# Small inverse beside the MLP in plain float32: two 94-column matmuls a job, and the split of v read from PSUM

## The reference

```
X = rfft(x, axis=1)                      # x: 4 x 3008 x 256
y = irfft(X * (filt_r + 1j*filt_i)[None], n=3008, axis=1)
x = y.reshape(12032, 256)
g = maximum(x @ moe_w_in, 0) ** 2        # 256 -> 2048
x = g @ moe_w_out                        # 2048 -> 256
gate = x @ moe2_w_gate; val = x @ moe2_w_val   # 256 -> 1536
out = (gate * sigmoid(gate) * val) @ moe2_w_out
```

## Time and profile before

| | |
|---|---|
| median of 3 runs | 2361.15 us (2359.8 to 2363.39) |
| profiled execution, its own time | 2358.64 us |
| its span | 2356.8 us |
| TensorE busy | 2329.5 us, 99% |
| VectorE busy | 1601.1 us, 68% |
| ScalarE busy | 1272.7 us, 54% |
| mean granted TensorE clock | 0.997 |

### The profile page before, as it was taken

The page is one execution under the profiler, slowest core; times in us unless marked ns, Lnnn a source line. Parts: engine busy times, 40 slices in busy tenths (PEclk is TensorE's granted clock), DMA queues, the critical chain, the costliest instruction groups (busy, mean ns, idle before and its releaser), DMA issues.

```text
span 2356.8 us, 31292 instructions
## 1 busy us (share of the span) xinstructions
PE 2329.5 (99%) x10581; PEld 1903.6 (81%) x10581; DVE 1601.1 (68%) x2707; ACT 1272.7 (54%) x2468; POOL 61.2 (3%) x124
## 2 busy tenths in 40 slices
PE   8899999999999999999999999999999999999999
PEld 4688888888888888888888878888888888888887
DVE  3567766677666776566555777777777777777776
ACT  4566656566655665555544445555555555555554
POOL 0100000000000000000000000000000000000000
PEclk9899999999999999999999999999999999999999
DMA  9643433333333333101002101001011011010000
GB/s 270 207 132 96 129 96 107 91 107 112 101 98 99 99 106 122 29 27 42 27 19 72 50 1 36 23 14 36 1 36 36 1 36 36 1 36 28 10 19 18
DMA packets 95423, 153.74 MB, mean 65 GB/s; under 512 B 10080, under 2 KB 48416, under 8 KB 94976
## 3 DMA queue, kind: packets, MB, share of 16 engines
q1 hardware_dynamic: 82112, 132.96, 17.9%
q0 software_dynamic: 13152, 18.78, 3.3%
HBM read 101.89 MB, written 49.81 MB: 64 GB/s over the span
## 4 chain that ended last, share of the span: by engine, by line
PE 96%; DMA 2%; SPq 1%; ACT 1%; issue 1%; DVE 1%; POOL 0%; ACTq 0%; DVEq 0%
PE psum L1450 31%; PE psum L1452 31%; PE psum L1451 31%; PE psum L1552 1%; DMA filt0b<-filt 1%; PE psum L1554 1%; PE psum L1461 1%; DMA B_scratch<-b_out 0%; SPq L562 0%; SPq L557 0%; PE psum L1504 0%; DMA w<-w_full 0%; ACT turned L820 0%; DMA A_scratch<-a_out 0%; ACT z_raw L820 0%
## 5 line engine op out<-in xcount | busy, mean ns | idle before, releaser
L1217 DVE SCALAR_TENSOR_TENSOR prod<-psum,act_out 128x512 f32<-128x512 f32 (+1 forms) x384 | 260.9, 679 | 398.4 <-ACT act_out L917 397.9
L917 ACT ACTIVATE act_out<-psum 128x512 f32<-128x512 f32 (+1 forms) x384 | 226.1, 589 | 461.5 <-PE psum L1452 461.2
L1450 PE MATMUL psum<-g_hi,m_hi 128*128 128x512 f32 (+1 forms) x768 | 305.7, 398 | 2.0 <-ACT z_raw L820 1.8
L1450 PE MATMUL psum<-v_hi,m_hi 128*128 128x512 f32 (+1 forms) x768 | 297.7, 388 | 1.5 <-DVE v_lo L1115 1.5
L1452 PE MATMUL psum<-v_hi,m_lo 128*128 128x512 f32 (+1 forms) x768 | 296.7, 386 | 0.0
L1451 PE MATMUL psum<-v_lo,m_hi 128*128 128x512 f32 (+1 forms) x768 | 296.7, 386 | 0.0
L1452 PE MATMUL psum<-g_hi,m_lo 128*128 128x512 f32 (+1 forms) x768 | 296.5, 386 | 0.0
L1451 PE MATMUL psum<-g_lo,m_hi 128*128 128x512 f32 (+1 forms) x768 | 296.4, 386 | 0.0
L1115 DVE TENSOR_TENSOR g_lo<-prod,g_hi 128x512 fp32r<-128x512 f32 (+1 forms) x408 | 270.6, 663 | 1.1 <-ACT g_hi L820 1.0
L820 ACT ACTIVATE g_hi<-prod 128x512 fp32r<-128x512 f32 (+1 forms) x408 | 248.5, 609 | 0.9 <-DVE prod L1251 0.9
L1450 PE MATMUL psum<-g_hi,m_out 128*128 128x512 f32 (+1 forms) x576 | 226.0, 392 | 0.3 <-DVE g_lo L1115 0.3
(11 more groups left out here) (125 smaller groups left out, 4246.9 us busy)
## 6 DMA issues: line engine op xcount, KB each, us to landing
filt_in<-filt SPq DMA_DIRECT2D x36, 512.0 KB, 3.9
z_scratch<-z_raw SPq DMA_DIRECT2D x23, 512.0 KB, 2.9
b_in<-B_scratch SPq DMA_DIRECT2D x122, 96.0 KB, 2.8
zq_raw<-z_scratch SPq DMA_DIRECT2D x44, 256.0 KB, 3.5
B_scratch<-b_out SPq DMA_DIRECT2D x38, 256.0 KB, 2.1
A_scratch<-a_out SPq DMA_DIRECT2D x50, 192.0 KB, 2.1
x_in<-x SPq DMA_DIRECT2D x48, 192.0 KB, 2.8
a_in<-A_scratch SPq DMA_DIRECT2D x36, 256.0 KB, 3.3
```

Of the source, the lines that this page charges most:

```text
L917: nc.scalar.activation(act_out[n % 2][:, 0:w], psum[:, n % 3, 0:w], ACT.Relu).then_inc(relu_done, 1)
L1217: nc.vector.scalar_tensor_tensor(out=prod[n % 2][:, 0:w], in0=psum[:, n % 3, 0:w], scalar=0.0, in1=act_out[n % 2][:, 0:w], op0=ALU.max, op ...
L1450: nc.tensor.matmul(dst, wh, vh, start=start, stop=False, skip_group_check=True)
```

## The change

The s4 job multiplies b as it was loaded with the table as it is, in plain float32: for each i one instruction with 94 columns. Its output in PSUM is the sum already, so copy_part, add_conv, the rings part and conv, and the splits of b go away; ScalarE's high_v reads PSUM and writes v_hi, VectorE's low_v reads PSUM and v_hi and writes v_lo, in the step of the job. Bank INV is free once v_lo is done. The ring of v holds three tiles instead of two, so a whole group is written at once, and only groups at the ring's end are in two pieces. load_b waits for s4 of two groups back instead of the split of that group, and the job itself waits for b's landing. w4's table is half as large. Tiles behind v in SBUF move by a few KB, and the blocks that hold the gated MLP's input are placed otherwise in the same region.

```diff
-RING = 2 * T
+RING = 3 * T
...
-    w4_full = w4[0:G0].transpose(2, 0, 1, 3)
-    w4 = halves(w4, 0).transpose(1, 3, 2, 0, 4)
+    w4 = w4.transpose(0, 2, 1, 3)
+    w4_full = w4[0:G0].transpose(1, 0, 2, 3)
...
-        b_hi, at = place_ring(at, "b_hi", 2, [ROWS, PAIR, D], F32R)
-        b_lo, at = place_ring(at, "b_lo", 2, [ROWS, PAIR, D], F32R)
-        w4, at = place_ring(at, "w4_", 2, [ROWS, PAIR, 2, Q], F32R)
-        part, at = place_ring(at, "part", 2, [P, GT])
-        conv_region = at
-        conv, at = place_ring(at, "conv", 2, [P, CH, GT])
-        fft_region = at
+        w4, at = place_ring(at, "w4_", 2, [ROWS, PAIR, Q])
...
+        at = fft_region = s4_region + 3 * CH * T * 4
...
-                wait(sp, b_lo_done, g - G0 - 1)
+                if g >= G0 + 2:
+                    sp.wait_ge(s4_done, s4_count(g - 2, CH - 1))
...
-            def high_b(g):
...
-            def copy_part(g, c):
...
-            def high_v(g, c, late):
-                t, col, src, size = v_spans(g)[late]
-                act.wait_ge(conv_done, s4_count(g, c))
-                if t >= 2:
-                    act.wait_ge(h_done, NF1 * (t - 1))
-                copy(v_hi[:, c, col:col + size], conv[g % 2][:, c, src:src + size]).then_inc(v_hi_done, 1)
+            def high_v(g, c):
+                act.wait_ge(s4_done, s4_count(g, c))
+                last = (GT * (g + 1) - 1) // T
+                if last >= 3:
+                    act.wait_ge(h_done, NF1 * (last - 2))
+                for col, lo, size in v_spans(g):
+                    copy(v_hi[:, c, col:col + size], psum[:, INV, lo:lo + size]).then_inc(v_hi_done, 1)
...
-            def low_b(g):
...
-            def add_conv(g, c):
...
+            def low_v(g, c):
+                dve.wait_ge(v_hi_done, v_count(g, c))
+                for col, lo, size in v_spans(g):
+                    low(v_lo[:, c, col:col + size], psum[:, INV, lo:lo + size], v_hi[:, c, col:col + size])\
+                        .then_inc(v_lo_done, 1)
...
                 if last_s4 is not None:
-                    pe.wait_ge(conv_done, s4_count(*last_s4))
+                    pe.wait_ge(v_lo_done, v_count(*last_s4))
...
-                pe.wait_ge(b_lo_done, g - G0 + 1)
+                pe.wait_ge(b_loaded[g % 2], 16 * PAIR * ((g - G0) // 2 + 1))
                 pe.wait_ge(w4_loaded[g % 2], 16 * ((g - G0) // 2 + 1))
                 wait(pe, b_copied, s3_jobs)
-                wait(pe, conv_done, s4_count(g, c) - 1)
-                dst = psum[:, INV, 0:2 * GT].rearrange("p (i h q) -> p i h q", i=PAIR, h=2)
+                pe.wait_ge(v_lo_done, v_count(g, 0) - len(v_spans(g)) if c == 0 else v_count(g, 0))
                 for i in range(PAIR):
-                    bh, bl = b_hi[g % 2][:, i, c * P:(c + 1) * P], b_lo[g % 2][:, i, c * P:(c + 1) * P]
-
-                    nc.tensor.matmul(dst[:, i, :, :], bh, w4[g % 2][:, i, :, :], start=True, stop=False,
-                                     skip_group_check=True)
-                    last = nc.tensor.matmul(dst[:, i, 0, :], bl, w4[g % 2][:, i, 0, :], start=False, stop=True,
-                                            skip_group_check=True)
+                    last = nc.tensor.matmul(psum[:, INV, Q * i:Q * (i + 1)], b_in[g % 2][:, i, c * P:(c + 1) * P],
+                                            w4[g % 2][:, i, :], start=True, stop=True, skip_group_check=True)
                 last.then_inc(s4_done, 1)
```

More of the change, by code:

```diff
@@ L181, in build @@
         b_in, at = place_ring(at, "b_in", 2, [ROWS, PAIR, D])
-        b_hi, at = place_ring(at, "b_hi", 2, [ROWS, PAIR, D], F32R)
-        b_lo, at = place_ring(at, "b_lo", 2, [ROWS, PAIR, D], F32R)
-        w4, at = place_ring(at, "w4_", 2, [ROWS, PAIR, 2, Q], F32R)
-        part, at = place_ring(at, "part", 2, [P, GT])
-        conv_region = at
-        conv, at = place_ring(at, "conv", 2, [P, CH, GT])
-        fft_region = at
+        w4, at = place_ring(at, "w4_", 2, [ROWS, PAIR, Q])
+        warm, at = place(at, "warm", [P, 2])
+        assert at <= s4_region + 3 * CH * T * 4
+        at = fft_region = s4_region + 3 * CH * T * 4
         x_in, at = place_ring(at, "x_in", 4, [QP, PAIR, D])
@@ L225, in build @@
         filt0a, at = place(v_region, "filt0a", [P, FILT0, 2, D])
-        assert at <= conv_region
+        assert at <= fft_region
         filt0b, at = place(a_hi_region, "filt0b", [P, K2 - FILT0, 2, D])
@@ L245, in build @@
         z_lo0, z_end = place(at, "z_lo0", [P, CH, T], F32R)
-        assert z_end <= fft_region
+        assert z_end == fft_region
         last_w = TOKENS - T * PLAIN[1]
@@ L251, in build @@
         a_raw, at = place(at, "a_raw", [P, 2 * CH, PIECE])
-        o_plain0, at = place(at, "o_plain0", [P, T])
-        assert at <= s4_region
+        o_plain0, o_plain0_end = place(at, "o_plain0", [P, T])
         z_in, z_hi, z_lo = [z_in0, z_in1], [z_hi0, z_hi1], [z_lo0, z_lo1]
@@ L259, in build @@
         BLOCK = 4 * T
-        blocks = [list(range(at, m1_end, BLOCK)) + list(range(z_end, fft_region - BLOCK + 1, BLOCK))
+        plain_end = v_region + 8 * BLOCK
+        assert plain_end >= o_plain0_end
+        blocks = [list(range(at, m1_end, BLOCK)) + list(range(plain_end, s4_region - BLOCK + 1, BLOCK))
                   + list(range(m2_end, room - BLOCK + 1, BLOCK)),
-                  list(range(v_region, z_end, BLOCK))]
+                  list(range(v_region, plain_end, BLOCK)) + list(range(s4_region, z_end, BLOCK))]
         zq_hi, zq_raw, zq_lo = [[], []], [[], []], [[], []]
@@ L344, in build @@
         b_copied = sem("b_copied")
-        b_hi_done = sem("b_hi_done")
-        b_lo_done = sem("b_lo_done")
         s4_done = sem("s4_done")
-        part_done = sem("part_done")
-        conv_done = sem("conv_done")
         v_hi_done = sem("v_hi_done")
@@ L455, in v_spans, with v_count, v_tile @@
             lo, hi = GT * g, GT * (g + 1)
[L456 to L466, removed]
+            edge = min(hi, RING * (lo // RING + 1))
+            return [(s % RING, s - lo, e - s) for s, e in ((lo, edge), (edge, hi)) if e > s]
+        def v_count(g, c):
+            if g < G0:
+                return CH
+            return CH * (1 + sum(len(v_spans(h)) for h in range(G0, g))) + (c + 1) * len(v_spans(g))
+        def v_tile(t):
+            return v_count(first_group(t + 1) - 1, CH - 1)
         def m2_at(n):
@@ L667, in load_z @@
                 if t == 0:
-                    sp.wait_ge(v_lo_done, v_count[TILES - 1])
+                    sp.wait_ge(v_lo_done, v_tile(TILES - 1))
                     sp.wait_ge(s4_done, s4_count(GROUPS - 1, CH - 1))
@@ L684, in load_zq @@
                     sp.wait_ge(g_used, STEPS)
-                    sp.wait_ge(conv_done, s4_count(GROUPS - 1, CH - 1))
                 elif k == 1:
@@ L802, in load_w4 @@
                     pool.wait_ge(s4_done, s4_count(g - 2, CH - 1))
-                pool.dma_start(w4[g % 2][:, :, :, :], w4_table[g % PGS, :, :, :, :]).then_inc(w4_loaded[g % 2], 16)
+                pool.dma_start(w4[g % 2][:, :, :], w4_table[g % PGS]).then_inc(w4_loaded[g % 2], 16)
             for u in range(UPS - 2):
@@ L823, in _ @@
             act.wait_ge(warm_ready, 1)
-            nc.scalar.activation(conv[0][:, 0, 0:1], conv[0][:, 0, 1:2], ACT.Sigmoid)
+            nc.scalar.activation(warm[:, 0:1], warm[:, 1:2], ACT.Sigmoid)
             def copy_a0(j):
@@ L882, in high_w_out @@
                 copy(m1_hi[:, W_IN + n, :], m1_raw[:, W_IN + n, :]).then_inc(m1_hi_done, 1)
-            def high_b(g):
[L885 to L888, removed]
-            def copy_part(g, c):
-                act.wait_ge(s4_done, s4_count(g, c))
[L892 to L895, removed]
-            def high_v(g, c, late):
-                t, col, src, size = v_spans(g)[late]
-                act.wait_ge(conv_done, s4_count(g, c))
-                if t >= 2:
-                    act.wait_ge(h_done, NF1 * (t - 1))
-                copy(v_hi[:, c, col:col + size], conv[g % 2][:, c, src:src + size]).then_inc(v_hi_done, 1)
+            def high_v(g, c):
+                act.wait_ge(s4_done, s4_count(g, c))
+                last = (GT * (g + 1) - 1) // T
[3 more added lines that the diff above has]
+                    copy(v_hi[:, c, col:col + size], psum[:, INV, lo:lo + size]).then_inc(v_hi_done, 1)
             def high_m2(w):
@@ L1033, in _ @@
                 if job is not None:
[L1034 to L1042, removed]
+                    high_v(*job)
                 u = s3_at(n)
@@ L1048, in _ @@
                     copy_a(j)
-                g = s4_group_at(n + 2)
-                if g is not None:
-                    high_b(g)
                 if n % 4 == 2 and n // 4 + 1 < W_IN // 2:
@@ L1115, in low @@
                 return nc.vector.tensor_tensor(dst, full, as_f32(hi), ALU.subtract)
-            nc.vector.memset(conv[0][:, 0, 1:2], 0.0).then_inc(warm_ready, 1)
+            nc.vector.memset(warm[:, 1:2], 0.0).then_inc(warm_ready, 1)
```

(12 more changed lines are left out.)

## The result

The changed kernel takes 2337.56 us (2336.49 to 2337.73, 4 runs) against 2361.1; the ratio is 0.9898, 95% interval 0.9881 to 0.9915. It is faster by 1.0%, outside the predicted range. Its profiled execution has a span of 2335.9 us, 20.9 less than before.

A forecast was written before the change was run, and what follows sets the result against it. TensorE, busy 99% of the span, was taken as the bound. Gains of 1.2 us (s4 jobs), 0.6 (start) and 0.2 (other waits) sum to 2.0, so 2361.15 becomes 2359.2 us; range 2353.5 to 2366.

The forecast's parts named there:

- What is costed at nothing: Changed bank release, engine and load waits, and later stages' new addresses: all priced at no time.
- the faster one (2345): Rival in the s4 jobs: loads hide, streaming sets the price at 346 ns a job, 15.4 us less; chance 0.05.
- The price of an s4 job: On TensorE, exposed weight loads set a job's cost: 470 ns instead of 480.
- the 30 ns for the long matmuls to fall back into their rhythm: Part of each s4 job's price on TensorE: some 30 ns lost after its short matmuls, before and after the change.
- the 1.2 us that I counted: Gain on TensorE from 115 s4 jobs not covered by waits for z, 10 ns each.
- The start: Ahead of the first x product: without b_lo, x_lo starts earlier and TensorE's 1.92 us wait shrinks by 0.60 us.
- The waits costed at nothing: Waits for the s4 and s3 bank, h_done, loads of b and w4, and b's landing: covered, no cost.
- my 0.2: Further shrinking of TensorE's 2.55 us of waits in the s4 stage, booked at 0.2 us, bounds 0 and 0.4.
- Draining between formats: Rival: array empties between s4's plain passes and float32r matmuls around them, 43.5 us slower, 2402; chance 0.07.
- loads that don't follow the clock: Rival: s4's plain loads stay at 212 ns at full clock, 34.3 us slower, 2394.7; chance 0.05.
- four loads a matmul: Rival: four passes per s4 matmul, eight loads a job instead of four, 50 us slower, about 2410; chance 0.03.
- the loads hide: Rival in the s4 jobs: streaming, not loads, sets the price, 15.4 us less, 2345; chance 0.05.

The follow-up runs named there:

- e1: Kernel before, s4 untouched, with only the region behind the s4 tiles starting 640 bytes later; 2337.33 us, ratio 0.9906 to the kernel before.
- e2: Changed kernel with the second MLP's weights, and the tiles over and behind them, moved by 1408 bytes to their old remainder; 2358.05 us, ratio 0.9995.
- e3: Changed kernel with only the three zq blocks behind the second MLP's weights moved by 1408 bytes; 2340.89 us, one run.
- e5: Changed kernel with every tile moved by 1408 bytes together, w4_0 laid over z_raw; 2332.75 us in one run, 2336.73 us when repeated.
- e6: Changed kernel with the second MLP's weights, and what lies over and behind them, moved by 512 bytes; 2338.87 us, single run.
- e11: Changed kernel with the second MLP's weights, and what lies over and behind them, moved by 32 bytes; 2359.18 us, single run.
- e4: Changed kernel with everything behind the first MLP's weights moved by 1408 bytes, w4_0 laid over z_raw; 2374.45 us.
- e12: Changed kernel with the first MLP's lo weights and the streamed v_lo and g_lo all moved by 128 bytes; 2352.19 us.
- e14: Changed kernel with only the first MLP's lo weights (m1_lo) moved by 128 bytes; 2349.48 us.
- e7: Changed kernel with the second MLP's weights, and what lies over and behind them, moved by 128 bytes; 2356.85 us, single run.
- e10: Changed kernel with the second MLP's weights, and what lies over and behind them, moved by 64 bytes; 2361.91 us, single run.

## Why the prediction was wrong

**The step that failed** is the last sentence of "What is costed at nothing": "The later stages only get other addresses." I gave it no price and no reason. Other addresses were worth 20.2 of the 20.9 us of the span in the quads alone (e1, e2), and the 1.0 us between z and the quads too: that stretch takes 93.3 to 93.6 us in every profile with the second MLP's weights out of step and 92.4 to 92.6 in every other. None of my rivals held it, and the faster one (2345) expected its gain in the s4 jobs, where none was. The trace of before had the hint: 231.3 ns a matmul in the quads against 226.7 in the first MLP for the same shape at the same clock, a difference that no wait and no instruction explained, and that I did not look at because TensorE counted as busy in both.

**The price of an s4 job held, but for its rhythm.** I had 470 ns after 480. The loads inside a job follow each other as those before did. In the timeline of loads of the changed kernel the row of the four plain loads begins at 1029.06, under the last long matmul; the second of them starts at 1029.283 and the float32r load behind the fourth at 1029.617, so the three exposed ones take 111 ns each, and the float32r load 113:

```profile
1029.06 0.64 PEld L1495 LDWEIGHTS psum<-w,b_in 96*128 96x128 f32 x4
1029.62 0.19 PEld L1396 LDWEIGHTS psum<-g_hi,m_hi 128*128 128x128 f32 x1
1029.73 0.19 PEld L1397 LDWEIGHTS psum<-g_lo,m_hi 128*128 128x128 f32 x1
```

So a plain float32 load at full clock lies within my bounds (106 to 112.5), a little above the 109 I took, and at about half of the 212 ns that it took at the granted clock 0.50. The steps, to be held against the earlier trace rows:

```profile
1027.92 0.39 PE L1396 MATMUL psum<-v_hi,m_hi 128*128 128x512 f32 x1
...
1031.11 0.40 PE L1396 MATMUL psum<-v_hi,m_hi 128*128 128x512 f32 x1
...
1033.85 0.39 PE L1396 MATMUL psum<-v_hi,m_hi 128*128 128x512 f32 x1
```

The step of the job takes 3.19 us, as predicted, but the pure one behind it 2.74 instead of 2.72: together 5.93 against 5.92. It is so throughout. The median of the 113 steps that hold an s4 job and nothing else went from 3.200 to 3.193 us, and the mean of the 64 pure steps right behind one from 2.730 to 2.741. The exposed loads are hardly cheaper (111 ns against 112.5), and the 30 ns for the long matmuls to fall back into their rhythm were too few: with 21 ns of the next step a job costs 494 ns, which leaves some 47 for it. This is the term of the job's price that was mis-sized, and the 1.2 us that I counted are not there. e1 gives the purest comparison, old s4 at the good placement: from its first x product (91.45, after a wait of 2.29) to z (1260.43) it takes 1168.98 us, the changed kernel 1169.64.

```profile
91.45 0.33 PE L1450 MATMUL psum<-x_hi,w 96*96 96x256 f32 x1 [2.29 <-DVE x_lo L1115]
...
1260.43 0.47 PE L1450 MATMUL psum<-z_hi,m_hi 128*128 128x512 f32 x1 [0.27 <-issue]
```

The eleven other profiles with the new s4 and the first MLP placed as in the changed kernel take 1169.5 to 1169.9. So the two instructions save no time of TensorE; they cost 0.5 to 0.9 us more than in e1, of which there is one profile. 244 instructions are 488 loads and 488 matmuls, as I expected from the rows of s4_0:

```profile
L1495 PEld LDWEIGHTS psum<-w,b_in x488: 187/191/192, 95.3 to 1208.5; 96*128 96x128 f32 x163
L1495 PE MATMUL psum<-w,b_in x488: 244/274/275, 95.6 to 1208.6; 96*128 96x94 f32 x163
```

**The start held in its mechanism, and the figure was lucky.** The wait ahead of the first x product went from 1.92 to 1.33 us, 0.59 where I had 0.60, and VectorE runs no b_lo ahead of x_lo any more. But the wait differs from run to run: e1, which still splits b, waited 2.29 us, and other runs of the new s4 waited 1.03 to 1.34. The product itself began at 93.42, not near 92.25, since the whole start ran late in that execution (first s4_0 matmul at 79.05 against 77.45).

**The waits costed at nothing held.** TensorE waits 2.40 us of the window from 95 to 1223 (1128.00 less 1125.60) against 2.55, my 0.2. The split of v has 138 pieces with the two of the start, as counted. VectorE fell to 66% and ScalarE to 52%, where I had 64 and 51, and neither mattered: I had multiplied durations that overlap, such as 0.62 us for instructions that start 0.52 apart.

**The rivals.** Draining between formats, loads that don't follow the clock, and four loads a matmul are refuted by the same rows: a job costs 0.47 us in its own step and 0.02 in the next. That the loads hide falls too: they stand 111 ns apart. The Trainium skill (FP8 and Floating Point Precision, TensorE Precision Notes) speaks of four passes; the trace has two loads and two matmuls for each instruction.

**What is shown and what is not.** Shown: moving weights alone, streamed tiles alone, or everything together changes or keeps the rate as their distance modulo 256 bytes does (e2, e3, e5, e6 to e11) in the gated MLP. In the first MLP the rate fell as well (e4, e12 to e14), but only distances that leave 128 were tried there, so its period is not shown. Not shown either: which two reads meet. e12 to e14 exclude both simple pairings, and whether successive loads, successive streams or a mixture count stays open.

s2 and s3 gained from the padding as well. Between e1 and the kernel before, the stage of the first MLP differs by 0.88 us, and the spacings inside, ahead of and behind the s2 and s3 jobs make up 0.86 of it; inside s2 they went from 230.6 to 227.0 ns. Their own weights and streamed tiles lay a multiple of 2048 bytes apart in both kernels. What changed is their distance to the first MLP's tiles, which stand around them: here too a neighbour out of step counts, as in e3. In the comparison of before with after, this gain hides what the new s4 costs.

## What to carry to other kernels

When a change alters the size of a tile, write down which tiles behind it move, and treat their new remainders modulo 256 bytes as part of the change; try the padding alone before crediting the edit. Compare the nanoseconds per matmul of equal shape between stages at equal clock: a stage that is slower without any wait is a finding, even where the engine counts as busy. Count weight loads, not instructions, when matmuls are short.

## What the runs showed of the hardware that I had not expected

In the gated MLP a float32r matmul of 512 columns came every 226.5 ns at best and every 231.3 to 232.2 ns with weights 32, 64 or 128 bytes off the streamed tiles' remainder modulo 256. The Trainium skill (TensorE: Matmul & The Clock Gate, Step-by-step: what each phase is for) says that TensorE has two independent read ports and that loading the next weights doesn't steal bandwidth from the running matmul. The runs speak against full independence in this use: in e2, e7, e10 and e11 nothing but the weights' address moved (with the output tiles laid over them and three blocks, two of them of zq), and the whole stage slowed by 2% or more. They do not say whether it is these two ports that meet.
